# Fused dynamic convolution and two feed-forward layers in fp32 on one core: a new order of the head and of the fill

## What is computed

```python
# 1. dynamic convolution: softmax over 7 taps, 8 heads of 24 channels
w = weight_gen - max(weight_gen, -1); w = exp(w); w = w / (sum(w, -1) + 1e-9)
x = einsum('bshk,bskhg->bshg', w, the 7 last tokens of x)
# 2. layer 1, with w_in 192 x 2048 and w_out 2048 x 192
h = x @ w_in
g = (a0 + a1*h + a2*h**2 + a3*h**3) / (1 + |b0|*|h| + |b1|*h**2 + 1e-6)
x = g @ w_out
# 3. layer 2, its own w_in and w_out
h = x @ w_in
y = (h * clip(h + 3, 0, 6) / 6) @ w_out
```

## Time and profile before

| | |
|---|---|
| median of 3 runs | 1256.51 us (1256.05 to 1257.59) |
| the profiled execution | 1257.45 us, of which its span 1255.6 |
| busy in the span | PE 1194.7 (95%), DVE 1182.0 (94%), ACT 1177.5 (94%), POOL 1108.0 (88%) |
| mean DMA rate | 61 GB/s |

### The profile page before, as it was taken

The page is one execution under the profiler, slowest core; times in us unless marked ns, Lnnn a source line. Parts: engine busy times, 40 slices in busy tenths (PEclk is TensorE's granted clock), DMA queues, the critical chain, the costliest instruction groups (busy, mean ns, idle before and its releaser), DMA issues.

```text
span 1255.6 us, 19215 instructions
## 1 busy us (share of the span) xinstructions
PE 1194.7 (95%) x5140; PEld 971.0 (77%) x5140; DVE 1182.0 (94%) x1902; ACT 1177.5 (94%) x2214; POOL 1108.0 (88%) x873
## 2 busy tenths in 40 slices
PE   2766999999999999999999999999999999999998
PEld 1544788888888888888888888888888888888876
DVE  6999999999999999999999999999999999999932
ACT  4888999999999999999999999999999999999954
POOL 5899799898999999899998989999898989966654
PEclk9788999999999999999999999999999999999999
DMA  8654033223312332321332233122323211000000
GB/s 215 143 133 78 19 76 69 55 51 79 72 37 65 65 70 51 75 61 39 79 63 55 51 86 64 39 70 58 63 51 85 51 43 43 17 18 13 6 17 13
DMA packets 62661, 76.58 MB, mean 61 GB/s; under 512 B 16152, under 2 KB 42520, under 8 KB 62040
## 3 DMA queue, kind: packets, MB, share of 16 engines
q1 hardware_dynamic: 61352, 73.40, 25.8%
q0 software_dynamic: 1200, 1.97, 1.4%
HBM read 57.49 MB, written 9.98 MB: 54 GB/s over the span
## 4 chain that ended last, share of the span: by engine, by line
POOL 34%; PE 34%; issue 22%; DVE 5%; ACT 2%; DMA 1%; SPq 0%; POOLq 0%; DVEq 0%; ACTq 0%
POOL g_lo L646 11%; POOL g_lo L637 9%; POOL mix L609 6%; POOL mix L616 5%; PE h L704 4%; PE h L707 3%; PE h L708 3%; PE h L706 3%; PE h L705 3%; PE acc L718 3%; PE acc L721 3%; PE acc L715 3%; PE acc L711 3%; PE acc L712 3%; DVE early L1176 1%
## 5 line engine op out<-in xcount | busy, mean ns | idle before, releaser
L637 POOL TENSOR_TENSOR g_lo<-early,g_hi 128x512 fp32r<-128x512 f32 x256 | 336.4, 1315 | 76.3 <-ACT g_hi L936 64.3
L646 POOL TENSOR_TENSOR g_lo<-late,g_hi 128x512 fp32r<-128x512 f32 x256 | 336.8, 1317 | 19.9 <-ACT g_hi L959 19.9
L704 PE MATMUL h<-x_hi,w_in_hi 128*128 128x512 f32 x512 | 206.0, 402 | 30.0 <-DVE early L1200 27.2
L1208 DVE SCALAR_TENSOR_TENSOR late<-late,h 128x512 f32<-128x512 f32 x256 | 176.1, 688 | 46.4 <-ACT late L947 43.6
L718 PE MATMUL acc<-g_lo,w_out 128*128 128x512 f32 x512 | 200.5, 392 | 4.8 <-DVE w_in_tail L1149 2.6
L711 PE MATMUL acc<-g_hi,w_out 128*128 128x512 f32 x512 | 200.8, 392 | 1.4 <-ACT late L997 0.8
L707 PE MATMUL h<-x_tail_hi,w_in_tail 128*128 128x512 f32 x512 | 201.8, 394 | 0.0
L705 PE MATMUL h<-x_lo,w_in_hi 128*128 128x512 f32 x512 | 201.7, 394 | 0.0
L706 PE MATMUL h<-x_hi,w_in_lo 128*128 128x512 f32 x512 | 201.6, 394 | 0.0
L721 PE MATMUL acc<-g_lo,w_out 128*128 128x512 f32 x512 | 200.5, 392 | 1.1 <-POOL g_lo L637 1.1
L708 PE MATMUL h<-x_tail_lo,w_in_tail 128*128 128x512 f32 x512 | 201.5, 394 | 0.0
(11 more groups left out here) (103 smaller groups left out, 2400.2 us busy)
## 6 DMA issues: line engine op xcount, KB each, us to landing
mix_w<-mix_weights SPq DMA_DIRECT2D x75, 192.0 KB
mix_w<-mix_weights SPq DMA_DIRECT2D x75, 144.0 KB
x_win<-in_x SPq DMA_DIRECT2D x15, 393.0 KB, 3.4
mix_w<-mix_weights SPq DMA_DIRECT2D x60, 96.0 KB
mix_w<-mix_weights SPq DMA_DIRECT2D x60, 72.0 KB
out_y<-late SPq DMA_DIRECT2D x16, 256.0 KB, 2.1
x_tail_hi<-tail_hi SPq DMA_DIRECT2D x60, 64.0 KB, 2.0
x_tail_lo<-tail_lo SPq DMA_DIRECT2D x60, 64.0 KB, 2.0
```

The source lines that it names most:

```text
L637: nc.gpsimd.tensor_tensor(g1_lo[p][:, :], neg_g[p], g1_hi[p][:, :].bitcast(F32), ALU.subtract).then_inc(g1_lo_ready, 1)
L646: nc.gpsimd.tensor_tensor(g2_lo[p][:, :], gate[p], g2_hi[p][:, :].bitcast(F32), ALU.subtract).then_inc(g2_lo_ready, 1)
L704: pe.matmul(out[:, :], w_hi[:, cols], hi[:, :], start=True, stop=False)
```

## The change

What it does, in order of the diff:

- `mix_weights` in DRAM becomes one tensor per part, [taps, 128, tokens], so that a part is stored by one DMA instead of eight; the loads read the same values.
- x of block 0 comes in two loads, rows 0 to 4 and rows 5 to 9, each with its own semaphore, both issued before part 0's load.
- SP issues part 1's load, w_out of layer 1 (first half) and x of block 1 before it waits for part 0's scale and stores part 0. The load of layer 2's w_in waits for GpSimd's four splits.
- Part 0's softmax moves: maximum on VectorE behind the row mixing, subtraction, seven sum steps and scale on GpSimd between the splits of w_in, exp on ScalarE behind the copies of x, reciprocal on VectorE behind the rests of x. `exp_gen(1)` moves into step 1.
- GpSimd makes the rests of all four quarters of layer 1's w_in (steps 1 and 2 for quarters 2 and 3); TensorE's copies and VectorE's splits of these fall away.
- The transposes wait for one add less ahead of the first four; the opening product (`first_of_all`) waits before each matmul for its operand, w_lo x_hi is taken before w_hi x_lo.
- New tables for mixing, weights and part 1, and for part 2's softmax.

```diff
-    mix_weights = nc.dram_tensor("mix_weights", [H, K, TOKENS], F32, kind="Internal").ap()
+    mix_weights = [nc.dram_tensor(f"mix_weights{part}", [K, P, part_tokens(part)], F32, kind="Internal").ap()
+                   for part in range(PARTS)]
...
-        PRODUCT_STEPS_1 = {2: (0,), 3: (1,), 6: (2,), 7: (3,), 8: (4,), 9: (5,), 11: (6,)}
-        ADD_STEPS_1 = {5: (1,), 7: (2,), 8: (3,), 9: (4,), 11: (5,), 13: (6,)}
-        PRODUCT_STEPS_2 = {0: (0, 1,), 1: (2,), 2: (3,), 4: (4,), 5: (5,), 8: (6,)}
-        ADD_STEPS_2 = {1: (1,), 2: (2,), 4: (3,), 5: (4,), 7: (5,), 12: (6,)}
+        PRODUCT_STEPS_1 = {4: (0, 1,), 6: (2,), 7: (3,), 8: (4,), 10: (5,), 11: (6,)}
+        ADD_STEPS_1 = {5: (1,), 7: (2,), 8: (3,), 10: (4,), 11: (5,), 12: (6,)}
+        PRODUCT_STEPS_2 = {0: (0, 1,), 1: (2,), 3: (3,), 5: (4,), 6: (5,), 9: (6,)}
+        ADD_STEPS_2 = {1: (1,), 3: (2,), 4: (3,), 6: (4,), 8: (5,), 12: (6,)}
...
-        IN_HI = {1: ((0, 2),), 3: ((0, 3),), 7: ((1, 0),), 8: ((1, 1),), 14: ((1, 2),), 16: ((1, 3),)}
-        TAIL_HI = {2: ((0, 2),), 3: ((0, 3),), 5: ((1, 0), (1, 1),), 7: ((1, 2),), 8: ((1, 3),)}
-        OUT_HI = {2: ((0, 0),), 4: ((0, 1), (0, 2),), 6: ((0, 3),), 9: ((1, 0),), 11: ((1, 1),), 15: ((1, 2),), 17: ((1, 3),)}
-        OUT_LO = {2: ((0, 0),), 6: ((0, 1),), 7: ((0, 2), (0, 3),), 13: ((1, 0), (1, 1),), 18: ((1, 2),), 20: ((1, 3),)}
-        SUM_1, RECIP_1, SCALE_1 = 1, 2, 3
+        IN_HI = {11: ((1, 0),), 14: ((1, 1),), 16: ((1, 2),), 17: ((1, 3),)}
+        TAIL_HI = {5: ((1, 0),), 6: ((1, 1), (1, 2),), 7: ((1, 3),)}
+        OUT_HI = {0: ((0, 0),), 2: ((0, 1),), 5: ((0, 2), (0, 3),), 8: ((1, 0),), 13: ((1, 1),), 15: ((1, 2),), 18: ((1, 3),)}
+        OUT_LO = {0: ((0, 0),), 4: ((0, 1),), 8: ((0, 2),), 10: ((0, 3),), 12: ((1, 0),), 18: ((1, 1), (1, 2),), 19: ((1, 3),)}
+        EXP_1, SUM_1, RECIP_1, SCALE_1 = 1, 1, 2, 4
+
+        IN1_HI = {1: (2,), 2: (3,)}
+        IN1_LO = {1: (2,), 2: (3,)}
...
             def store_gen(part):
-                n = part_tokens(part)
-                start = part_blocks(part)[0] * BLOCK
-                for hd in range(H):
-                    dst = mix_weights[hd, :, start:start + SUB * n].rearrange("k (s n) -> s k n", s=SUB)
-                    sp.dma_start(dst, gen_w(part)[hd * SUB:(hd + 1) * SUB, :, :]).then_inc(gen_stored[part], 16)
+                sp.dma_start(mix_weights[part].rearrange("k p n -> p k n"), gen_w(part)).then_inc(gen_stored[part], 16)
...
             sp.dma_start(w_rows, gen_head[:, :]).then_inc(w_rows_loaded, 16)
+            for i, rows in enumerate(X_LOADS):
+                sp.dma_start(x_rows[:, rows, :], x_head[:, rows, :]).then_inc(x_rows_loaded[i], 16)
             load_gen(0)
-            sp.dma_start(x_rows, x_head[:, :, :]).then_inc(x_rows_loaded, 16)
...
-            sp.wait_ge(gen_scaled, 1)
-            store_gen(0)
             load_gen(1)
             sp.dma_start(w_slot(out_slot[0]), w_half(w_out1, 0)).then_inc(out1_staged[0], 16)
             load_x(1)
+            sp.wait_ge(gen_scaled, 1)
+            store_gen(0)
...
-            sp.wait_ge(in1_lo, 2)
-            sp.wait_ge(lo_split, split_count(0, 3))
+            sp.wait_ge(in1_lo, 4)
             sp.dma_start(in_slot, w_in2[0:P, :]).then_inc(in2_staged, 16)
...
             split_in1(0)
+            subtract_max(0)
+            split_in1_tail(0)
+            for k in range(1, K + 1):
+                sum_tap(0, k)
             split_in1(1)
+            scale(0)
+            split_in1_tail(1)
             subtract_max(1)
...
-            pe.wait_ge(rows_mixed, ROW_STEPS)
...
             for part, out in enumerate((h2, h1[2])):
+                pe.wait_ge(rows_mixed, ROW_STEPS - 1 + part)
...
+            def first_of_all():
+                out, (hi, lo, tail_hi, tail_lo) = h1[0], x1[0]
+                pe.wait_ge(x1_first_hi, 1)
+                pe.matmul(out[:, :], w_in_hi[0][:, 0:P], hi[:, :], start=True, stop=False)
+                pe.wait_ge(in1_lo, 1)
+                pe.matmul(out[:, :], w_in_lo[0][:, 0:P], hi[:, :], start=False, stop=False)
+                pe.wait_ge(x1_first_lo, 1)
+                pe.matmul(out[:, :], w_in_hi[0][:, 0:P], lo[:, :], start=False, stop=False)
+                pe.wait_ge(x1_first_hi, 2)
+                pe.wait_ge(in1_tail_lo, 1)
+                pe.matmul(out[:, :], w_in_tail[0][:, 0:P], tail_hi[:, :], start=False, stop=False)
+                pe.wait_ge(x1_first_lo, 2)
+                pe.matmul(out[:, :], w_in_tail[0][:, 0:P], tail_lo[:, :], start=False, stop=True).then_inc(h1_ready, 1)
...
-            for i in (0, 1):
-                round_in(0, i)
-                round_tail(0, i)
+            round_in(0, 0)
+            round_in(0, 1)
+            round_tail(0, 0)
             act.wait_ge(x1_turned, 1)
             act.copy(x1[0][0][:, :], h2).then_inc(x1_first_hi, 1)
             act.wait_ge(x1_turned, 2)
             act.copy(x1[0][2][:, :], h1[2]).then_inc(x1_first_hi, 1)
-            exp_gen(1)
+            exp_gen(0)
+            round_tail(0, 1)
...
-            max_gen(0)
             dve.wait_ge(rows_exp, 1)
...
             linked(6, dve.tensor_tensor(w, w, row_wide, ALU.mult))
-            sum_gen(0)
...
+            max_gen(0)
             dve.wait_ge(x1_first_hi, 1)
             dve.tensor_tensor(x1[0][1][:, :], h2, x1[0][0][:, :].bitcast(F32), ALU.subtract).then_inc(x1_first_lo, 1)
             dve.wait_ge(x1_first_hi, 2)
             dve.tensor_tensor(x1[0][3][:, :], h1[2], x1[0][2][:, :].bitcast(F32), ALU.subtract).then_inc(x1_first_lo, 1)
+            recip_whole(0)
             max_gen(1)
```

More of the change, by code:

```diff
@@ L363, in sum_count @@
         def sum_count(part, k=K):
-            return 2 if part == 0 else 2 + K * (part - 1) + k
+            return K * part + k
         def recip_count(part, half=1):
@@ L404, in load_mix_w @@
             def load_mix_w(blk, taps, loaded):
+                part = blk // 2
+                at = (blk - part_blocks(part)[0]) * BLOCK
+                by_head = mix_weights[part].rearrange("k (h s) n -> h k (s n)", h=H)
                 for head, row, rows, token, tokens, col in MIX_ROWS:
-                    src = mix_weights[head, taps, bass.ds(count(BLOCK, blk, token), tokens)]
+                    src = by_head[head, taps, at + token:at + token + tokens]
                     sp.dma_start(mix_w[row:row + rows, taps, col:col + tokens],
@@ L570, in split_in1 @@
             def split_in1(i):
-                cols, rows = fourth(F, i), lo_rows(0, i)
+                cols = fourth(F, i)
                 pool.wait_ge(in_hi[0], i + 1)
@@ L673, in prepare @@
                     n = (s + 1) * NC + c
+                    for i in IN1_LO.get(n, ()):
+                        split_in1(i)
+                        split_in1_tail(i)
                     for m, i in OUT_LO.get(n, ()):
@@ L1007, in prepare @@
                     n = (s + 1) * NC + c
+                    for i in IN1_HI.get(n, ()):
+                        round_in(0, i)
+                        round_tail(0, i)
                     for m, i in IN_HI.get(n, ()):
@@ L1013, in prepare @@
                         round_out(m, i)
+                    if n == EXP_1:
+                        exp_gen(1)
                     for part, _ in part_steps(s, "exp", c):
@@ L1073, in max_fourth, with recip_whole @@
                                   ALU.max).then_inc(gen_max, 1)
+            def recip_whole(part):
+                dve.wait_ge(gen_sum, sum_count(part))
+                dve.reciprocal(gen_stat(part), gen_stat(part)).then_inc(gen_recip, 1)
             def recip_half(part, half):
```

54 lines of the change are left out of this document (24 added, 30 removed).

## The result

The change makes the kernel slower: 1259.61 us median of 8 runs (1258.54 to 1263.85) against 1255.86 of the 8 runs of before beside it (1254.88 to 1257.59), a ratio of 1.0036 with a 95% interval of 1.0025 to 1.0046. That is 3.75 us more, where 0.9 us less was forecast. The profiled execution of after is the longest of the eight, 1263.85 us with a span of 1261.8; where its lines say more than the median bears out, a second and a third profiled execution of the same kernel stand beside it (spans 1260.7 and 1258.1).

What follows compares the result with a forecast made beforehand. The fill before about 130 us, a loop of VectorE, ScalarE and TensorE with GpSimd nearly full, was taken as the bound. Gains of 2.4 and 0.3 less 1.3 and 0.5 made 0.9 us: 1255.6 us median, range 1251.5 to 1260.5.

Steps and rivals of the forecast that it cites:

- The likeliest case: Whole kernel: 0.9 us gained, median 1255.6 us, within 0.2% (1254.0 to 1259.0); chance 0.46.
- GpSimd becomes the bound: Rival, block 1's fill: mix weights at 39.5 us and late second loads overload GpSimd; 3.5 us slower, 1260 us, chance 0.18.
- What bounds the kernel: Time won or lost before about 130 us reaches the end unchanged; after that TensorE is full and nothing gains.
- The head up to the transposes: Opening of block 0: VectorE starts on x at 5.85 instead of 6.95 us, transposes start at 15.2.
- The same bytes lie ahead of that load as before, so it lands at 16.5 again: Head: the tail of layer 1's w_in lands at 16.5 us, unchanged; the first product ends 3.0 us sooner.
- What VectorE gives back: Before chunk 0: VectorE's wait for part 1's sum costs 1.0 of 3.0 us; chunk 0 starts at 22.3, gaining 2.0.
- The mix weights come later: Block 1's mix weights land at 38.1 us, not 32.6; VectorE waits 3.7 us and chunk 5's gain falls to 0.4.
- Chunk 6 starts at 51.7: Chunk 5, with a tail round and two w_out rounds on ScalarE, puts chunk 6 at 51.7 against 51.42: 0.3 us lost.
- Chunk 12 and what follows: Chunks 6 to 12 take 26.8 us, chunk 12 gaining 2.4; two more splits in chunks 12 to 18 cost 1.3.
- The sum: Chunk 22, where TensorE becomes full: 2.4 - 1.3 - 0.5 + 0.3 = 0.9 us gained.
- The weights come in time: Rival, block 1's mix weights: landing by 36.5 us or no VectorE wait gives 4.0 us gain, 1252.5 us; chance 0.36.
- The head does not move: Rival, head: w_in1's tail lands 1.5 us or more later, chunk 0 gains only 0.5; 1257 us, chance 0.05.

Runs made afterwards that it cites:

- loads held back: The changed kernel with SP waiting for the tail of layer 1's w_in before issuing the loads behind it: 1259.6 us, ratio 1.0036.
- part 0 early, one x: The changed kernel with part 0's softmax and the store's old order back in the head, and x in one load: 1252.0 us, ratio 0.9971.
- g_lo first: The changed kernel with tap 1's product and w_out's first split one step later, so g_lo of chunk 1 follows one product: 1260.58 us, ratio 1.0035.
- SP's order: The changed kernel with block 2's mix weight loads issued ahead of SP's wait for layer 1's last w_out split: 1259.33 us, ratio 1.0023.
- loads in the gap: The changed kernel with w_out1's second half and the tail of layer 2's w_in issued before the wait for part 0's scale: 1262.04 us, ratio 1.0049.

## Why the prediction was wrong, point by point

The time lies inside the range, near its upper end, but the sign is wrong. The likeliest case, no measurable change, put the sum at 0.9 us of gain. That 1259.6 lay inside was luck: the range reached it only by the rival of 1260, whose mechanism was at most partly the one at work.

- **What bounds the kernel: right.** Whatever is lost or won before TensorE is full is carried to the end: the span less the start of chunk 27 is 1105.5 to 1105.8 us in the seven columns of the table.
- **The head up to the transposes: right.** Row products start at 5.52 (5.85 forecast), the transposes at 14.95 (15.2).
- **"The same bytes lie ahead of that load as before, so it lands at 16.5 again": this step failed.** It landed at 22.0 to 22.3 in three profiled executions of after, and chunk 0 started 5.0 us later than forecast. The same bytes came at another rate. What brings this about in after is x in two loads: with x in one load the tail was back at 18.33 and 16.61 and the time 2.8 us lower (1259.61 - 1256.82). In the kernel before the split alone costs 2.0 us, and 0.5 of the 1.2 us by which w_in is later there is that SP issues one DMA more ahead of it (3.54 instead of 3.07). The step rested on counting bytes and looked at no row for what it costs to cut a load in two; its bound of "1 us late" was taken from nothing. The prediction leaned here on the Trainium skill ("DMA: Bandwidth & Descriptors", Queues, rings and completion order), which says that each DMA engine consumes the descriptors in ring order. With one x the trace agrees: in the second profiled execution the loads behind the tail were issued from 5.2 us and it landed at 16.61. But the order did not fix the time: with the same order of loads the tail landed at 17.53 in one kernel and at 21.98 in another.
- **What VectorE gives back: right.** It waits 1.86 us for GpSimd's sum ahead of chunk 0, and where the tail landed at 17.02, chunk 0 started at 22.34 (22.3 forecast).
- **The mix weights come later: right.** Scale ends to weights landed was put at 15.1 us (23.0 to 38.1). In after the scale ends at 28.24 (27.56 + 0.68) and the weights are there at 43.35: 15.1. With the loads held back the scale ends at 23.25 and the weights are there at 38.12.
- **"Chunk 6 starts at 51.7": this step failed too.** From chunk 5 it took 7.3 us in after and 7.6 with the loads held back, against 5.0. The forecast moved twelve mix loads by 11.6 us (18.83 to 30.42) and did not follow what is issued behind them: the tail of layer 2's w_in, issued at 35.75, landed at 54.56. ScalarE's round of it was moved to step 5 by the new table; in the kernel before it came at 47.92 and waited for nothing. It is the rule that was followed for GpSimd and forgotten for SP: of a moved step every DMA behind it moves too.
- **Chunk 12 and what follows.** From chunk 6 to 12 it took 26.4 us in after (59.01 to 85.39), where 26.8 was forecast and before took 29.5: right. Chunks 12 to 16 took 19.3 us against 16.6 of before, where 1.3 more were foreseen up to chunk 18; the wait for `x_tail_lo` is 2.7 of it, but it comes and goes between executions. "Loads issued at 50" was wrong: SP waited 7.2 us for the landing of part 1's store, issued at 49.80 into a full queue, and issued them at 57.41.
- **The sum.** For the profiled execution, against the forecast starts: +5.0 at chunk 0 (27.32 for 22.3), +5.0 at chunk 5, +7.3 at chunk 6, +6.9 at chunk 12 and +7.3 at the end (1263.85 for 1256.55). The first failed step thus makes 5.0 of it and the second 2.3; that execution is 4.2 us over the median. For the medians: late part 0 costs 4.8 (1256.82 - 1252.0), splitting x 2.8 (1259.61 - 1256.82), and all the rest gains 3.6 (by the ratio 0.9971) to 4.6 (by the medians, 1256.57 - 1252.0). These are the steps of one path from before to after by way of two kernels, so that they add up to some 3.75 is no check of them; in another order of the steps they are other numbers (6.9 for late part 0, 0.7 for the split). With one x the change as a whole comes to 0.5 us slower (ratio 1.0007 [0.9998, 1.0017]): without the first failed step no change could have been told, as the likeliest case said, though not the gain of its sum.
- **The rivals.** "The weights come in time" fell; its 1252.5 is near the 1252.0 measured where they were in time (part 0 early, one x). Against the 1255.6 of the likeliest case that makes the late weights cost 3.1 us, where 4.5 to 5.1 were measured. "GpSimd becomes the bound" was to decide once the second loads are issued after 53, and they were, at 57.41; but ScalarE did not wait for w_out2 in chunk 8, as it said it would. "The head does not move" was right that the tail is over 1.5 us late, and at 1257 too mild: it had the tail stop chunk 0 from gaining, not lose 3 us.
- **What stays open.** Why the queue moved 167 to 248 GB/s between 10 and 20 us in four executions (after in all three, g_lo first) and 265 to 286 in two others (SP's order, loads in the gap) with the same loads in the same order was not settled, nor why x in two loads should make the slow one likelier. Held back or not, the median with two loads was 1259.6; but the slow one was seen only where SP did not wait ahead of the loads behind w_in. So their early issue is neither shown to matter nor ruled out. Nor is it shown why splitting x costs less with part 0 early.

The best of the kernels run keeps the new head, splits and tables, loads x at once and makes part 0 before the rows are mixed: 1252.0 us, 4.57 under the 1256.57 beside it.

## What to carry to other kernels

When a producer of a small DMA is moved off one path, write down the whole queue behind its load, in order, with who waits for each item: here three engines depended on what stood behind it, and where one wait was removed, another took its place. Test a late chain by bringing its source forward before you shorten its links: the source was worth 4.8 us, and no link that was shortened here lowered the time. And before a load is cut in two to have its first half sooner, measure the cut by itself: it won 0.5 to 1.2 us on the rows (they start at 5.52, with one x at 6.01 to 6.70) and cost 2 to 3 us in all where part 0 is late or the kernel is that of before.
